# Scores of an attention pair directly behind the product of the pair ahead, and the last two expert tiles' maxima one after the other

## What is computed

```python
# 1: windowed attention, 8 heads of 64
scores = scale * q @ k.T ; masked to a window of 32 (heads 0-3)
                           or a dilated window of 128, step 4 (heads 4-7)
attn = softmax(scores) ; x = attn @ v                 # (B, 576, 512)
# 2: gated two-layer product, x_prev = x one token back
xk = mu_k * x + (1 - mu_k) * x_prev ; xr likewise with mu_r
k = max(xk @ w_k, 0) ; v = (k * k) @ w_v ; r = sigmoid(xr @ w_r)
x = r * v
# 3: four causal attention experts of width 64, the best two per token
w = softmax over the two largest of x @ w_gate
out += w_e * softmax(causal((x wq_e) @ (x wk_e).T)) @ (x wv_e) @ wo_e
```

## Time and profile before

| | |
|---|---|
| median of 3 runs (lowest, highest) | 547.62 us (547.53, 549.23) |
| the profiled execution | 548.58 us |
| its span, first to last instruction | 546.8 us |
| busy: PE, DVE, ACT, POOL | 97%, 61%, 49%, 42% |
| mean granted TensorE clock | 0.994 of full speed |
| chain that ended last | PE 77%, ACT 7%, DVE 7%, POOL 5% |

### The profile page before, as it was taken

The page is one execution under the profiler, slowest core; times in us unless marked ns, Lnnn a source line. Parts: engine busy times, 40 slices in busy tenths (PEclk is TensorE's granted clock), DMA queues, the critical chain, the costliest instruction groups (busy, mean ns, idle before and its releaser), DMA issues.

```text
span 546.8 us, 12317 instructions
## 1 busy us (share of the span) xinstructions
PE 531.0 (97%) x5042; PEld 474.5 (87%) x5042; DVE 335.3 (61%) x687; ACT 267.7 (49%) x692; POOL 230.0 (42%) x285
## 2 busy tenths in 40 slices
PE   7899898999999999999999999999999999999997
PEld 6789898998669999999767989999976899999765
DVE  4779959713588983930468895672247785630461
ACT  5788464223764534423484553432267463322484
POOL 7667765321354651431254554233044564230250
PEclk9899999999999999999999999999999999999999
DMA  8993110210003202201002120100000200000002
GB/s 298 341 347 96 46 40 39 78 34 1 2 24 109 63 17 78 62 18 34 2 1 88 46 78 1 34 2 1 2 2 1 86 2 1 2 1 1 1 1 88
DMA packets 8935, 29.62 MB, mean 54 GB/s; under 512 B 1200, under 2 KB 1200, under 8 KB 8880
## 3 DMA queue, kind: packets, MB, share of 16 engines
q1 hardware_dynamic: 6256, 24.12, 14.0%
q10 hardware_dynamic: 2624, 4.72, 2.7%
HBM read 24.12 MB, written 4.72 MB: 53 GB/s over the span
## 4 chain that ended last, share of the span: by engine, by line
PE 77%; ACT 7%; DVE 7%; POOL 5%; issue 1%; DMA 1%; SPq 0%; POOLq 0%; DVEq 0%; ACTq 0%
PE MM L568 21%; PE MM L570 19%; PE MM L569 19%; PE OA L556 3%; PE TR L719 2%; PE OA L742 2%; PE TR L541 2%; ACT c_prob L931 2%; PE SC L691 2%; PE SC L525 2%; POOL k_lo L1422 1%; ACT c_probT L944 1%; PE MM L691 1%; DMA raw_wr_lo<-in_w_r 1%; DVE c_negmax L1266 1%
## 5 line engine op out<-in xcount | busy, mean ns | idle before, releaser
L1422 POOL TENSOR_TENSOR k_lo<-ring,k_hi 128x288 fp32r<-128x288 f32 x64 | 55.8, 874 | 79.0 <-ACT k_hi L908 79.0
L1450 POOL TENSOR_SCALAR c_prob<-c_prob,c_inv,gates 128x512 f32<-128x512 f32 (+3 forms) x64 | 38.6, 612 | 100.3 <-DVE c_inv L1276 100.3
L568 PE MATMUL MM<-k_hi,wv_hi 128*128 128x288 f32 x256 | 76.2, 298 | 3.0 <-POOL wv_lo L1459 1.9
L568 PE MATMUL MM<-act_hi,wk_hi 128*128 128x288 f32 x256 | 77.5, 303 | 0.1
L569 PE MATMUL MM<-k_lo,wv_hi 128*128 128x288 f32 x256 | 75.5, 295 | 0.0
L569 PE MATMUL MM<-act_lo,wk_hi 128*128 128x288 f32 x256 | 75.3, 294 | 0.0
L570 PE MATMUL MM<-k_hi,wv_lo 128*128 128x288 f32 x256 | 75.3, 294 | 0.0
L570 PE MATMUL MM<-act_hi,wk_lo 128*128 128x288 f32 x256 | 75.2, 294 | 0.0
L1208 DVE RECIPROCAL gate_r<-gate_r 128x288 f32<-128x288 f32 x32 | 62.5, 1953 | 1.1
L1161 DVE SCALAR_TENSOR_TENSOR mix<-xT,one_less,mix 128x288 f32<-128x288 f32 x64 | 51.7, 811 | 8.9 <-ACT mix L1020 8.0
L568 PEld LDWEIGHTS MM<-k_hi,wv_hi 128*128 128x128 f32 x256 | 48.0, 187 | 3.9 <-POOL wv_lo L1459 2.1
(11 more groups left out here) (189 smaller groups left out, 1381.5 us busy)
## 6 DMA issues: line engine op xcount, KB each, us to landing
qkT<-in_qk SPq DMA_DIRECT2D x16, 591.5 KB, 3.8
vn<-in_v SPq DMA_DIRECT2D x16, 432.0 KB, 4.6
out_x<-c_prob ACTq DMA_DIRECT2D x16, 224.0 KB, 2.3
raw_wk_lo<-in_w_k SPq DMA_DIRECT2D x4, 512.0 KB, 16.5
raw_wv_lo<-in_w_v SPq DMA_DIRECT2D x4, 512.0 KB, 18.5
raw_wr_lo<-in_w_r SPq DMA_DIRECT2D x2, 512.0 KB, 8.2
out_x<-c_prob ACTq DMA_DIRECT2D x4, 256.0 KB, 2.0
raw_cv_lo<-in_c_v SPq DMA_DIRECT2D x1, 520.0 KB, 17.7
```

Source lines behind the costliest of these rows:

```text
L568: nc.tensor.matmul(dst, w2[0], x2[0], start=first, stop=False)
L1422: nc.gpsimd.tensor_tensor(lo, ring[:, ITEM[u] % RING, :], hi.bitcast(fp32), ALU.subtract)\
L1450: nc.gpsimd.tensor_scalar(prob_tile(u), prob_tile(u), c_inv[:, u:u + 1], gate, ALU.mult, ALU.mult).then_inc(c_prob, 1)
```

## The change

Two edits. The first moves SCORE and EXP of the first attention one step forward, to offsets 1 and 2; SOFT, TURN and APPLY keep theirs. Since APPLY is at offset 9 and a pair is 8 steps, the scores of pairs 1 to 3 then fall into the step of the product of the pair ahead and stand directly behind it. The second moves, on VectorE in the expert part, the maximum of the tile k = 3 ahead of the sum of tile k = 2.

```diff
-        return [(p, i - PER_PAIR * p) for p in range(PAIRS) if 2 <= i - PER_PAIR * p < 10]
+        return [(p, i - PER_PAIR * p) for p in range(PAIRS) if SCORE <= i - PER_PAIR * p <= APPLY]
...
-    SCORE, EXP, SOFT, TURN, APPLY = 2, 3, 4, 7, 9
+    SCORE, EXP, SOFT, TURN, APPLY = 1, 2, 4, 7, 9
...
             for k in range(1, PAIR_TILES):
-                for u in TILE_UNITS[k]:
-                    dve_c_max(dve, b, u)
+                if k != BOTH_LAST[1]:
+                    for u in TILE_UNITS[k]:
+                        dve_c_max(dve, b, u)
+                if k == BOTH_LAST[0]:
+                    for u in TILE_UNITS[BOTH_LAST[1]]:
+                        dve_c_max(dve, b, u)
```

## The result

| | before | changed |
|---|---|---|
| median of 7 runs each (lowest, highest) | 549.23 us (547.53, 550.01) | 546.46 us (544.63, 547.01) |
| ratio, 95% interval | | 0.9944 (0.9926 to 0.9962) |
| the profiled execution | 548.58 us | 546.74 us |
| its span | 546.8 us | 544.9 us |
| mean granted TensorE clock | 0.994 | 0.997 |

By the ratio the changed kernel is faster by 0.56%, 3.1 us (2.1 to 4.1) of the 549.23; the two medians themselves are 2.8 us apart. The forecast was a gain of 3.8 us, and 543.8 us (542.0 to 546.0) as the median: the sign holds and the size is near, but the median lies 0.5 us above the range. Two things are in that miss: a term of 1.2 us that did not come, and a base that was too low (547.62 in three runs, 549.23 in seven).

A forecast was written before the change was run, and what follows sets the result against it. TensorE was busy 97% of the span, leaving only its waits and small losses between instructions. Terms of 1.4 + 1.2 + 1.2 = 3.8 us off 548.58 gave 544.8, less 0.96 for the median: 543.8 us (542.0 to 546.0).

The forecast's parts named there:

- Transitions: First attention, pairs 1 to 3: scores directly behind the product save 0.20 us at seven places, 1.4 us (0.7 to 1.8).
- The wait for u11's low half: First v unit: earlier VectorE and ScalarE work removes 0.6 of TensorE's 0.66 us gap in two batches, 1.2 us (0.7 to 1.3).
- Maxima in a row: Experts: earlier maximum brings the second last tile's turn 0.31 us forward in four batches, 1.2 us (0 to 1.6).
- Rival C: Most is taken back: experts' turn waits for GpSimd anyway, only five transitions remain; 1.0 us gain, 546.6 us; chance 0.10.
- Batch 0: First batch: no gain or loss counted, since its large waits hang on weight halves made one after another.
- The gate's wait: Start of batch 0: TensorE newly waits about 1 us for u3's gate, hidden by the later wait for GpSimd's weight half.
- The turn of pair 2: Batch 0 at 89.88 us: its 1.5 us wait stays, as four VectorE and GpSimd weight halves run one after another.
- rival A: Batch 0: GpSimd starts its weight half ahead of VectorE's, shrinking TensorE's longest gap; 542.7 us; chance 0.18.
- The base: Starting time: 548.58 us profiled execution, then 0.96 us taken off because the median of the runs was 547.62.

The follow-up runs named there:

- EXP at 3: Changed kernel with scores still a step earlier (offset 1) but the exponential back at offset 3; 546.05 us, 0.9946 of before.
- pair 0 late: Changed kernel with pair 0's scores and exponential back at steps 2 and 3, pairs 1 to 3 moved; 546.62 us, 0.9952 of before.
- steps only: Changed kernel with the experts' maxima put back in their old order, scores and exponentials still a step earlier; 545.89 us, 0.9943 of before.
- cut product: Changed kernel with the experts' product of tile k = 1 split, part ahead of the turn of k = 2, the rest behind; 545.73 us, 0.9942 of before.
- halves at 28 and 29: Changed kernel with GpSimd's low halves of expert weights cv and ck moved late in batch 0, from steps 16 and 17 to 28 and 29; 546.67 us, 0.9957.
- both together: Changed kernel with the experts' product of tile k = 1 split around the turn of k = 2, and cv, ck halves at steps 28, 27; 543.84 us, 0.9918.
- first v half early: Changed kernel with GpSimd's low half of the first w_v quarter moved from step 6 to 3 of batch 0; 546.33 us, 0.9942 of before.
- maxima only: Changed kernel with SCORE and EXP put back to offsets 2 and 3, the experts' maxima still in a row; 549.03 us, 0.9999 of before.
- cut without maxima: Changed kernel with the experts' product of tile k = 1 split around the turn of k = 2, maxima in old order; 545.19 us, 0.9936 of before.
- halves at 28 and 27: Changed kernel with GpSimd's low halves of cv and ck moved from steps 16 and 17 to 28 and 27 of batch 0; 544.57 us, 0.9921.

## Why the prediction was right or wrong

*Transitions, 1.4 us: right.* 0.21 us at the place shown above, seven places. The step from product to scores costs what leaving the product always did. The Trainium skill, TensorEngine Tiling (Array Packing), section Key Properties, has a change of tiling mode drain TensorE, and I had read from it a saving of 0.10 only. The trace does not contradict the drain, since the new step is no cheaper than the old way out of the product. My count was right, one of five changes goes, but not every change costs 0.10: the way from product to dense unit costs 0.10 on the product's side and 0.11 on the dense unit's, the ones into the scores, old and new, about 0.10. So the one that goes is worth 0.21.

*The wait for u11's low half, 1.2 us: right.* 2 x 0.66 = 1.3, forecast 1.2. The low half ended at 195.91, within the 195.4 to 196.0 worked out, though that was on before's scale and the rows now lie 0.9 us later; on the same scale it was earlier than forecast. The run with EXP at 3 corrects the reason: the exponential's place did not matter, VectorE's order was enough. The earlier softmax of pair 0, which my working took as a help, was none either, as the run with pair 0 late shows.

*Maxima in a row, 1.2 us: wrong, and this is the step that failed.* It said "0 if another wait takes its place", and took 0.31 all the same. I had followed one chain back from the turn (scaling, sum, exponential, maximum) because the row named GpSimd. I did not ask when the other thing was ready that this turn needs, the banks it writes. The trace of before had the answer, in rows that I had passed over (ACT and POOL):

```profile
276.33 0.26 ACT L941 ACTIVATE c_probT<-TR 64x128 f32<-64x128 f32 x1
...
275.78 0.82 POOL L1450 TENSOR_SCALAR c_prob<-c_prob,c_inv,gates_last 128x576 f32<-128x576 f32 x1 [1.08 <-DVE c_inv L1276]
```

The copy out of those banks ended at 276.59, the scaling at 276.60, and the turn came at 276.74, 0.14 behind the copy as in all runs where the copy holds it. So even a scaling that ended at once would not have moved the turn. Hence 0 in every run without the cut, and 0.18 us a batch with it. Why I let it pass can be named: in the prediction "ScalarE copies turned tiles and then idles 0.31 us" speaks of the copies ahead of the exponential, not of those behind it, and "TensorE's gap is large enough to take it" measured the gap, not its causes. Rival C had this outcome (the turn waits all the same), but for GpSimd and bundled with the loss of the u11 term, at 0.10.

*Batch 0, 0: right in the result, and partly by luck.* The gate's wait came (0.85 for about 1) and cost nothing, but the weight half, named as its cover, covered only 0.17 us of it (1.87 against 2.04 us in the run with EXP at 3); the rest was paid by smaller waits ahead of it that went away, which I had not listed. The turn of pair 2 did not move. VectorE was ahead of GpSimd at 56.12 to 56.23, by 0.11 us, so rival A did not come. The Trainium skill, SBUF — State Buffer, section SBUF: two separate sides, has VectorE and GpSimd share an exclusive lock. The trace agrees: an instruction took 3.42 us beside GpSimd's and 1.22 in the run with late halves, where GpSimd makes none beside it. (The 1.1 us that I used for one alone is what such an instruction takes beyond the end of GpSimd's; a whole one takes 1.2.) But "stay where they are" I had treated as given. It was a wait that two numbers in a table remove, and worth 1.4 us, as much as all transitions.

*The base: wrong by 1.6 us.* The sum stood against 548.58 us and gave 544.8, inside the range and 1.7 under the result. I then took 0.96 us off because the three runs had a median of 547.62. With seven runs it was 549.23, and about 549.1 beside the other kernels (549.16, 548.96, 549.09). The three were not typical. Of the 42 executions of the kernel before beside the experiments, six had a mean clock of 1.000 and took 547.40 to 547.55 us; the other 36 took 547.76 to 551.79. Two of my three (547.53 and 547.62) look like the six; their clocks are not on record, so this stays an argument. As a ratio the forecast was 0.9930 and the measurement 0.9944 (0.9926 to 0.9962).

Terms corrected: 1.4 + 1.3 + 0 = 2.7 us; measured 3.1 (2.1 to 4.1). Of the 2.7 us between the forecast of 543.8 and the median of 546.46, the base makes 1.6. The other 1.0 is what the forecast gain of 3.8 us has over the 2.8 between the medians; the term that did not come explains that.

## What to carry to other kernels

When a wait is to be shortened through one of its causes, list all that the waiting instruction needs (its inputs, and the buffer it writes) with the time each was ready. The profile names only the last one, and two that end within 0.01 us look like one. If the buffer is freed by an engine that itself waits for the instruction before, the remedy is more work between the two, not a faster chain.

A weight half that nobody wants for 20 us, made beside one that lies ahead of a critical softmax, made that one two to three times as long here (2.02 and 3.42 us instead of 1.2). Move it to where its engine idles, in the order in which the halves are wanted, and look for the place where it is wanted next; at the wrong step the whole gain comes back as another wait.

Take the base from as many runs as the effect is small, and compare distances between like points of two traces before medians.

## What the runs showed of the hardware

The granted clock of TensorE fell to half of full speed (from 2.4 to 1.2 GHz) once or twice in each profiled execution, for 3.4 or 6.8 us (its last microseconds aside), and at one of three places, differing between executions of kernels that are alike there:

| half clock, us of the span | kernels |
|---|---|
| 11 to 19 | before, steps only, cut product, halves at 28 and 29, both together |
| 25 to 33 | pair 0 late, first v half early |
| 59 to 65 | changed, steps only, maxima only, EXP at 3, cut without maxima, halves at 28 and 27, both together |

Windows of the changed kernel, PE alone (window, its length, PE busy and instructions, granted clock, DMA share, GB/s):

```profile
57.00:60.00 3.00, 1.13 (x9) 1.00 0.00 0
60.00:66.00 6.00, 5.84 (x33) 0.72 0.00 0
```

of the run with the cut product:

```profile
57.00:60.00 3.00, 0.97 (x6) 1.00 0.00 0
60.00:66.00 6.00, 6.00 (x46) 1.00 0.01 3
```

and of before, at the start:

```profile
13.00:16.00 3.00, 2.50 (x37) 0.50 1.05 285
```

Each of the three places lies behind or among waits of TensorE: at the start for loads, at 57 us for the v half. But the same 2 us pause is followed by a stretch at half clock in the changed kernel and by none in the runs with the cut product and with pair 0 late, so the pause does not decide it alone; what does, no run here shows. The price differs by place. At 61 us TensorE has dense work, and its matmuls follow each other every 0.24 us instead of 0.133:

```profile
61.45 0.44 PE L568 MATMUL MM<-k_hi,wv_hi 128*128 128x288 f32 x1
61.69 0.44 PE L569 MATMUL MM<-k_lo,wv_hi 128*128 128x288 f32 x1
```

3.4 us of it cost 14 x 0.107 = 1.5 us, as the way to pair 2's turn confirms: 31.38 us from 59.62 in the changed kernel, 29.85 from 59.04 in the run with the cut product. At the start the loads fill their engines (a share of 1.05 above), and 3.4 us of it cost nothing that shows: the first dense product of batch 0 starts at 27.94 to 29.40 us with such a stretch and at 28.91 to 29.34 without one. A stretch of 6.8 us there goes with 29.56 and 30.85, and one of 6.8 us at 25 to 33 with 31.10 and 31.74, some 2 us later. The run with both edits has 3.4 us at the start and 3.4 at 59, and its span, 541.2 us, is the shortest. Of the seven timed executions of the changed kernel the one with a clock of 1.000 throughout took 544.63 us, those at 0.994 to 0.997 took 545.48 to 547.01. So the place of the stretch makes a good part of the scatter of the medians here, and a median of three executions can be off by 1.5 us when two of them miss the place at 59 to 65. That is as large as each term that I had argued about.
